# Attention on one core: shared block as two 64-column products, last rows padded to 128, products of one array shape issued together, low halves split a step later

## The reference

```python
def _attn_ref(q, k, v, tau):          # q, k, v: (4, 8, 576, 64) float32
    scale = 1.0 / np.sqrt(q.shape[-1])
    scores = scale * np.matmul(q, k.transpose(0, 1, 3, 2))
    thresh = np.max(scores, axis=-1, keepdims=True) - tau
    scores = np.where(scores >= thresh, scores, -1000000000.0)
    scores = scores - np.max(scores, axis=-1, keepdims=True)
    attn = np.exp(scores)
    attn = attn / (np.sum(attn, axis=-1, keepdims=True) + 1e-09)
    return np.matmul(attn, v).astype(np.float32)
```

## Time and profile before

| | |
|---|---|
| three runs | 1110.48, 1111.07, 1113.72 us; median 1111.07 |
| profiled execution | 1115.11 us; span of its instructions 1113.4 us |
| busy in the span | PE 94%, DVE 60%, ACT 50%, POOL 39% |
| attention part | to about 333 us of the span |
| TensorE's mean granted clock | 0.975 |

### The profile page before, as it was taken

How to read it: one execution, slowest core, us unless ns; L and a number is a source line. 1 busy time by engine, 2 the same in 40 slices (tenths; PEclk the granted TensorE clock), 3 DMA queues, 4 the chain that set the end, 5 groups by cost and what they waited for, 6 DMA issues and landing times. The chain is left out here.

```text
span 1113.4 us, 22407 instructions
## 1 busy us (share of the span) xinstructions
PE 1042.4 (94%) x8153; PEld 924.9 (83%) x8153; DVE 664.1 (60%) x1336; ACT 554.3 (50%) x854; POOL 432.9 (39%) x689
## 2 busy tenths in 40 slices
PE   7999999999989999999899989999379999999995
PEld 5778787787869999999899989999367777777774
DVE  5888787877855534343334333433567777777773
ACT  4777777777762311111111111111167888777772
POOL 4777777777750000000000000000147766667752
PEclk9999999999998999999999999999579999999998
DMA  4323223232203100000000000000782455511100
GB/s 107 80 60 82 53 66 80 63 81 51 53 2 115 39 20 1 25 1 20 3 25 1 20 2 24 1 20 1 277 322 112 166 197 183 190 38 39 39 28 22
DMA packets 76314, 75.40 MB, mean 68 GB/s; under 512 B 48815, under 2 KB 54959, under 8 KB 76210
## 3 DMA queue, kind: packets, MB, share of 16 engines
q1 hardware_dynamic: 72690, 63.49, 18.5%
q0 software_dynamic: 3520, 10.49, 2.8%
HBM read 64.52 MB, written 10.49 MB: 67 GB/s over the span
## 5 line engine op out<-in xcount | busy, mean ns | idle before, releaser
L820 ACT ACTIVATE r_buf<-h_ps 128x288 f32<-128x288 f32 x128 | 52.7, 412 | 348.2 <-PE h_ps L777 348.2
L884 DVE TENSOR_TENSOR r_buf<-r_buf 128x288 f32<-128x288 f32 x128 | 58.7, 459 | 244.4 <-ACT r_buf L820 244.4
L1156 POOL MEMSET ones<- 128x128 bf16 x1 | 0.2, 210 | 454.0 <-POOLq L637 454.0
L1322 ACT ACTIVATE w_hi<-w_experts 128x2048 fp32r x88 | 161.5, 1908 | 14.0 <-issue 14.0
L1093 DVE TENSOR_TENSOR w_lo<-w_experts,w_hi 128x2048 fp32r<-128x2048 f32 x66 | 149.5, 2292 | 28.0 <-ACT w_hi L1322 28.0
L777 PE MATMUL h_ps<-x_hi,w_in_hi 128*128 128x288 f32 x512 | 154.5, 302 | 6.6 <-DVE x_lo L878 3.5
L777 PE MATMUL h_ps<-x_hi,w_in_lo 128*128 128x288 f32 x512 | 151.9, 297 | 3.4 <-issue 3.4
L777 PE MATMUL h_ps<-x_lo,w_in_hi 128*128 128x288 f32 x512 | 152.5, 298 | 0.0
L796 PE MATMUL y_ps<-g_hi,w_out_hi 128*128 128x288 f32 x512 | 151.5, 296 | 0.3 <-DVE g_lo L890 0.3
L796 PE MATMUL y_ps<-g_hi,w_out_lo 128*128 128x288 f32 x512 | 151.3, 296 | 0.0
L796 PE MATMUL y_ps<-g_lo,w_out_hi 128*128 128x288 f32 x512 | 151.2, 295 | 0.0
(11 more groups left out here) (193 smaller groups left out, 2338.6 us busy)
## 6 DMA issues: line engine op xcount, KB each, us to landing
w_experts<-in_moe_w_dram SPq DMA_DIRECT2D x16, 2048.0 KB, 12.6
k_raw<-in_k_dram SPq DMA_DIRECT2D x32, 128.0 KB, 3.1
q_raw<-in_q_dram SPq DMA_DIRECT2D x32, 128.0 KB, 2.9
w_raw<-in_moe_w_in_dram SPq DMA_DIRECT2D x16, 256.0 KB, 3.2
v_nat<-in_v_dram SPq DMA_DIRECT2D x16, 256.0 KB, 2.6
y_T<-in_moe_w_out_dram SPq DMA_DIRECT2D x16, 256.0 KB, 2.7
y_rows<-y_row SPq DMA_DIRECT2D x16, 256.0 KB, 2.2
v_odd<-in_v_dram SPq DMA_DIRECT2D x16, 64.0 KB, 2.3
```

The costliest lines, as they stand in the source:

```text
L820: nc.scalar.activation(r_buf[f % 2][:], h_ps[f % 2][:, 0:HALF], ACT.Relu).then_inc(relu_done, 1)
L884: nc.vector.tensor_tensor(r[:], r[:], r[:], ALU.mult).then_inc(g_ops, 1)
L1156: nc.gpsimd.memset(ones[:], 1.0).then_inc(pool_set, 1)
L1322: nc.scalar.activation(group_of(w_hi, g), raw_group(buf, g), ACT.Copy).then_inc(hi_done, 1)
```

## The change

- The shared block is multiplied as two products of 64 columns (`v_mix[:, 0:D]` for the even head, `v_mix[:, D:2*D]` for the odd one), beside the four others: five pairs of half products and no full one.
- The last 64 rows are padded to 128: v's last rows lie in partitions 64 to 127 with zeros before them, k's last rows have zeros behind them, and the transposes and products of the tail and the ends use all 128 rows.
- `broadcast_rinv` (c = 1) and `output_tail` (now c = 3, one step later) are issued right behind `output_main`.
- The tail and the ends have columns of their own in `m_ps`; the wait for the tail's readers moves from `transposed_ends` to `transposed_k`.
- `q_hi` and `q_lo` move from c = 1 to c = 2, `ends_hi` and `ends_lo` from c = 3 to c = 4, the tail's copy and normalisation to c = 4. Orders within steps of ACT and DVE change with them; the reciprocal goes from the end of step 0 to behind the first maximum of step 1.

```diff
@@ attention: constants @@
+        SETUP = 12
+        TAIL_OUT, TAIL_R, Q_END, K_END = 0, TAIL, 2 * TAIL, 2 * TAIL + P
@@ load_v @@
-                sp.dma_start(v_nat[b][0:TAIL, :, LAST, :],
+                sp.dma_start(v_nat[b][TAIL:P, :, LAST, :],
@@ transposed_k @@
-                if i >= 1:
+                if i == 1:
+                    pe.wait_ge(klo_done, 1)
+                elif i >= 2:
                     pe.wait_ge(elo_done, 2 * i)
+                if i >= 3:
+                    pe.wait_ge(rbc_tail_done, i - 2)
+                    pe.wait_ge(x_tail_done, i - 2)
@@ transposed_ends @@
-                else:
-                    pe.wait_ge(rbc_tail_done, i - 1)
-                    pe.wait_ge(x_tail_done, i - 1)
-                pe.transpose(bank[:, 0:P], q_raw[b][:, LAST, :], ident[:])
-                pe.transpose(bank[:, P:P + TAIL], k_raw[b][0:TAIL, LAST, :], ident[0:TAIL, 0:TAIL]).then_inc(ends_set, 1)
+                pe.transpose(bank[:, Q_END:Q_END + P], q_raw[b][:, LAST, :], ident[:])
+                pe.transpose(bank[:, K_END:K_END + P], k_raw[b][:, LAST, :], ident[:]).then_inc(ends_set, 1)
@@ transposed_probs @@
-                    last = pe.transpose(out[0:TAIL, 0:P], probs[c][:, MAIN:S], ident[:])
+                    last = pe.transpose(out[:, 0:P], probs[c][:, S - P:S], ident[:])
@@ output_main @@
-                for kc in range(LAST):
-                    pe.matmul(o_ps[0:D, cols], v_nat[b][:, 0, kc, :], pt[:, kc, :], ...)
-                    pe.matmul(o_ps[D:P, cols], v_odd[b][:, kc, :], pt[:, LAST + 1 + kc, :], ...)
-                pe.matmul(o_ps[:, cols], v_mix[b][:], pt[:, LAST, :], start=False, stop=(c == LAST - 1),
-                          skip_group_check=True).then_inc(pv_done, 1)
+                for kc in range(QC):
+                    even = v_nat[b][:, 0, kc, :] if kc < LAST else v_mix[b][:, 0:D]
+                    odd = v_mix[b][:, D:2 * D] if kc == 0 else v_odd[b][:, kc - 1, :]
+                    pe.matmul(o_ps[0:D, cols], even, pt[:, kc, :], ...)
+                    last = pe.matmul(o_ps[D:P, cols], odd, pt[:, LAST + kc, :], ...)
+                last.then_inc(pv_done, 1)
@@ output_tail @@
-                    rows = P if kc < LAST else TAIL
-                        last = pe.matmul(m_ps[D * par:D * (par + 1), 0:TAIL], v_nat[b][0:rows, par, kc, :],
-                                  tail_T[0:rows, kc, par * TAIL:(par + 1) * TAIL], ...)
+                        last = pe.matmul(m_ps[D * par:D * (par + 1), TAIL_OUT:TAIL_OUT + TAIL], v_nat[b][:, par, kc, :],
+                                         tail_T[:, kc, par * TAIL:(par + 1) * TAIL], ...)
@@ TensorE's loop @@
-                if c == 1 and i >= 1:
-                    broadcast_rinv(i - 1)
                 if 0 <= made[0] < PAIRS:
                     for s in range(2):
                         transposed_probs(*made, s)
                 if c == 0 and i + 1 < PAIRS:
                     transposed_k(i + 1)
                 if 0 <= used[0] < PAIRS and used[1] < LAST:
                     output_main(*used)
+                if c == 1 and i >= 1:
+                    broadcast_rinv(i - 1)
+                if c == 3 and i >= 1:
+                    output_tail(i - 1)
                 if 0 <= made[0] < PAIRS and sets_in(made[1]) == 3:
                     transposed_probs(*made, 2)
                 if c == 1 and i + 1 < PAIRS:
                     transposed_q(i + 1)
-                if 0 <= used[0] and used[1] == LAST:
-                    output_tail(used[0])
                 if c == 3 and i + 1 < PAIRS:
                     transposed_ends(i + 1)
@@ ACT's copy_rinv_tail @@
+                if i + 2 < PAIRS:
+                    act.wait_ge(ends_set, i + 3)
@@ ACT's loop @@
+                if c == 2 and i + 1 < PAIRS:
+                    q_hi(i + 1)
+                if c == 4 and i >= 1:
+                    copy_rinv_tail(i - 1)
+                if c == 4 and i + 1 < PAIRS:
+                    ends_hi(i + 1)
                 if 0 <= made[0] < PAIRS:
                     for s in range(2):
                         evacuate(*made, s)
+                if c == 0 and i + 1 < PAIRS:
+                    k_hi(i + 1)
                 if i < PAIRS:
                     exponential(i, c, 0)
+                if c == 1 and i >= 1:
+                    copy_rinv(i - 1)
                 if 0 <= made[0] < PAIRS and sets_in(made[1]) == 3:
                     evacuate(*made, 2)
                 if i < PAIRS and len(heads_in(c)) == 2:
                     exponential(i, c, 1)
@@ DVE: setup @@
+                V.memset(v_nat[b][0:TAIL, :, LAST, :], 0.0).then_inc(setup_done, 1)
+                V.memset(k_raw[b][TAIL:P, LAST, :], 0.0).then_inc(setup_done, 1)
@@ DVE's loop, as it is after @@
+                if i < PAIRS:
+                    maximum(i, c, 0)
+                if c == 1 and i >= 1:
+                    reciprocal(i - 1)
+                if i < PAIRS and len(heads_in(c)) == 2:
+                    maximum(i, c, 1)
+                if c == 2 and i + 1 < PAIRS:
+                    q_lo(i + 1)
+                if c == 4 and i + 1 < PAIRS:
+                    ends_lo(i + 1)
                 if 0 <= before[0] < PAIRS:
                     for h in heads_in(before[1]):
                         mask(*before, h)
                 if c == 0 and i + 1 < PAIRS:
                     k_lo(i + 1)
+                if c == 2 and i >= 1:
+                    normalise_main(i - 1)
+                if c == 4 and i >= 1:
+                    normalise_tail(i - 1)
```

More of the change, by code:

```diff
@@ L383, in output_main @@
                     else:
-                        pe.wait_ge(setup_done, 8)
+                        pe.wait_ge(setup_done, SETUP)
                 pe.wait_ge(evac_done, set_no(i, c, 2) + 1)
                 pt, cols = probs_T[m % 2], slice(c * P, (c + 1) * P)
-                for kc in range(LAST):
[L388 to L391, removed]
-                pe.matmul(o_ps[:, cols], v_mix[b][:], pt[:, LAST, :], start=False, stop=(c == LAST - 1),
-                          skip_group_check=True).then_inc(pv_done, 1)
+                for kc in range(QC):
+                    even = v_nat[b][:, 0, kc, :] if kc < LAST else v_mix[b][:, 0:D]
+                    odd = v_mix[b][:, D:2 * D] if kc == 0 else v_odd[b][:, kc - 1, :]
+                    pe.matmul(o_ps[0:D, cols], even, pt[:, kc, :], start=(c == 0 and kc == 0),
+                              stop=(c == LAST - 1 and kc == LAST), skip_group_check=True)
+                    last = pe.matmul(o_ps[D:P, cols], odd, pt[:, LAST + kc, :], start=(c == 0 and kc == 0),
+                                     stop=(c == LAST - 1 and kc == LAST), skip_group_check=True)
+                last.then_inc(pv_done, 1)
             def broadcast_rinv(i):
@@ L416, in output_tail @@
                 for par in range(2):
-                    pe.matmul(m_ps[D * par:D * (par + 1), TAIL:2 * TAIL],
+                    pe.matmul(m_ps[D * par:D * (par + 1), TAIL_R:TAIL_R + TAIL],
                               rinv[:, CHUNKS - 1:CHUNKS].broadcast_to([P, D]),
@@ L420, in output_tail @@
                 for kc in range(QC):
-                    rows = P if kc < LAST else TAIL
                     for par in range(2):
-                        last = pe.matmul(m_ps[D * par:D * (par + 1), 0:TAIL], v_nat[b][0:rows, par, kc, :],
-                                  tail_T[0:rows, kc, par * TAIL:(par + 1) * TAIL], start=(kc == 0), stop=(kc == LAST))
+                        last = pe.matmul(m_ps[D * par:D * (par + 1), TAIL_OUT:TAIL_OUT + TAIL], v_nat[b][:, par, kc, :],
+                                         tail_T[:, kc, par * TAIL:(par + 1) * TAIL], start=(kc == 0), stop=(kc == LAST))
                 last.then_inc(tail_set, 1)
@@ L434, in _ @@
             scores(0, 0)
-            for step in range(STEPS * PAIRS + 3):
+            for step in range(STEPS * PAIRS + 4):
                 i, c = divmod(step, STEPS)
                 made, used = divmod(step - 2, STEPS), divmod(step - 3, STEPS)
-                if c == 1 and i >= 1:
-                    broadcast_rinv(i - 1)
                 if 0 <= made[0] < PAIRS:
@@ L470, in ends_hi @@
                 bank = qk_bank(i, "ends")
-                nc.scalar.activation(kT_hi[i % 2][:, MAIN:S], bank[:, P:P + TAIL], ACT.Copy).then_inc(ehi_done, 1)
-                nc.scalar.activation(qT_hi[i % 2][:, MAIN:MAIN + P], bank[:, 0:P], ACT.Copy, scale=SCALE).then_inc(ehi_done, 1)
+                nc.scalar.activation(kT_hi[i % 2][:, MAIN:S], bank[:, K_END:K_END + TAIL], ACT.Copy).then_inc(ehi_done, 1)
+                nc.scalar.activation(qT_hi[i % 2][:, MAIN:MAIN + P], bank[:, Q_END:Q_END + P], ACT.Copy,
+                                     scale=SCALE).then_inc(ehi_done, 1)
             def exponential(i, c, h):
@@ L493, in evacuate @@
                 else:
-                    out, src = tail_T[0:TAIL, LAST, :], src[0:TAIL, 0:P]
+                    out, src = tail_T[:, LAST, :], src[:, 0:P]
```

(14 more changed lines are left out.)

28 lines of the change are left out of this document (4 added, 24 removed).

## The result

The changed kernel takes 1120.87 us in the median of five runs, the kernel before 1111.07: a ratio of 1.0084, with a 95% interval of 1.0060 to 1.0108. I had forecast 1114.7 in a range of 1107 to 1122, slower with a chance of 0.50.

The account below looks back on a forecast made before the run. TensorE's queue was taken to bound the attention, other engines close behind. Savings of 1.2 us a pair against stalls of 0.87 and 0.64 left +0.33 a pair, +3.6 us overall: 1114.7 from 1111.07, range 1107 to 1122.

Parts of the forecast that it names:

- Stall A: At transposed_q in step 1: TensorE waits for ACT's copy of the reciprocal broadcast, 0.87 us, 14 times.
- Stall B: Second transpose set of step 3: TensorE waits for DVE's masks of chunk 1, queued behind q_lo, 0.64 us a pair.
- step 3: 4.82: Time from the start of scores 3 to scores 4, forecast to grow from 3.86 to 4.82 us.
- Wait C: Step 0: TensorE waits for a bank because POOL's bias for chunk 4 is late; 0.07 us, between 0 and 0.3.
- Savings by shape: TensorE, per pair: shared block 0.22, broadcast behind output_main 0.15 plus 0.22 waiting, tail 0.33, ends 0.28; 1.2 us together.
- The rival that the shape price is not saved: Transposes ahead of scores still pay an entry and 128-row tails cost more: +0.2 to 0.5 a pair, 1118 to 1122; chance 0.07.
- steps 4 and 0: Times from scores 4 to the next scores 0, and from scores 0 to scores 1: forecast 3.36 and 4.00 us.
- The sum: 20.04 against 19.71 us a pair, +0.33, x14 = +4.6; first pair -0.1, last pair -0.9; +3.6 us.
- The weight load: Load behind load_v on SP's queue might reach POOL late; mostly slack supposed, otherwise 1119 to 1124, chance 0.13.

Follow-up runs that it names:

- Experiment 5: The changed kernel with broadcast_rinv, its copy and the reciprocal back at their old places, all else kept; ratio to the kernel before 1.0006.
- Experiment 2: The changed kernel with normalise_main moved from the end of DVE's step 2 to the end of its step 1; ratio to the kernel before 1.0046.
- Experiment 3: The changed kernel with DVE's step 2 reordered to maxima, masks, normalisation, then q_lo; ratio to the kernel before 1.0088.
- experiment 7: The kernel before with the last rows padded to 128 and every order as before; ratio to the kernel before 0.9982.
- experiment 8: The kernel before with the padding alone and POOL's weight split of step 3 moved behind the biases of step 4; ratio to the kernel before 0.9951.
- experiment 4: The changed kernel with normalise_main at the end of DVE's step 1 and q_lo behind the masks in step 2; ratio to the kernel before 0.9962.
- experiment 9: The kernel before with padding, POOL's split moved a place later, and the shared block as two halves; ratio to the kernel before 0.9921.

## Why the prediction was right, and where it was short

- *Stall A*: right. The transposes start 1.74 after the broadcast's first record (I had 1.85), so the stall is 0.76 where I had 0.87; the profile puts 9.8 us of idle time on this wait. Taking it away gave 1.35 a pair: the 0.76, and 0.59 for the transposes, which now fill the masks' wait. Experiment 5 shows the stall from the other side: with its cover back, 0.37 less a pair in spite of one block more.
- *Stall B*: right in place, cause and size (second set at S2 + 4.67; step 3 shorter by 0.60 once the masks come first).
- *The step that failed* is the term "step 3: 4.82". I named the normalisation as queued behind the masks, and looked for who waits for DVE after it (the maxima of chunk 3), but not for who waits for the normalisation itself: `output_main` of chunk 0 needs `x_main_done`. Experiment 2 gives this wait 0.17 a pair. The other 0.14 of step 3 (5.13 less 4.82) no run takes apart; in the trace it is several small terms: the tail with its exit takes 0.82 (145.47 to 146.29) where I had 0.75, the transposes and the ends behind it 0.53 (146.29 to 146.82) where I had 0.50, the second set starts 0.02 later and takes 0.02 more, and I had rounded 4.84 to 4.82.
- *Wait C* was priced at 0.07 and did not occur in the changed kernel: step 0 is 3.95, 0.04 shorter than before. Experiment 3, where step 3 is 0.60 shorter and the wait appears, fits with step 3's length having covered it. The mechanism is real: 0.73 in experiment 3, 0.50 in experiment 7, gone in 8.
- *Savings by shape*: right in sign and kind, too high in what reaches the time. The shared block gives 0.12 of 0.22, block and padding together 0.47 of some 0.7. Part of the difference is price: in steps 3, 4 and 0 the shared block gives 0.04 each, not 0.055, and the padded tail 0.14, not 0.19. Part is cover: in step 1 the reciprocal takes the block's 0.04, and in step 3 of experiment 8 `output_main` starts 1.89 after S3 instead of 1.78, its transposes in the masks' wait, while the ends save 0.26 of the 0.28. The rival that the shape price is not saved would give the same time as measured (1118 to 1122), but not these steps: in the changed kernel steps 4 and 0, which have no stall, came out at 3.35 and 3.95 where I had 3.36 and 4.00.
- *The sum*: 14 x 0.20 more a pair is 2.8 us, and 3.6 + 2.8 is 6.4; the attention really ends 6.3 later. The rest, 2.2 us of the profiled executions and 3.5 us of the medians, lies in parts that the change does not touch, and the twelve traces show it with either kernel. That the loss came out clear of noise, and not on its edge as forecast, is owed to step 3 and to these parts together.
- *The weight load*: today's slack took it, as supposed. In the changed kernel it was waited for only twice, for 0.9 us in all between 40 and 300 us.

## What to carry to other kernels

Putting products of one shape together saves a fixed price a block, but each of them also carries a hand-over (a bank, a copy) whose cover was the work that stood between. List for every moved instruction who waits for it, not only what it waits for. When TensorE's step gets shorter, look at once at the chains of the small engines with the next smallest slack; an order that puts off-path work where its engine is idle can be worth as much as the shapes: here moving the normalisation and `q_lo` took 0.77 a pair (experiment 4), the shapes alone 0.47 (experiment 9). And where a wait has two possible causes, look at which of them ended last, with its usual delay, before believing the name beside it.

## What the runs showed of the hardware

A POOL subtraction of 128x128 took 0.46 us when it started before one of DVE's masks, and 0.97 to 0.99 when it started inside one; the mask behind it then took 1.00 to 1.01 instead of 0.81. In the kernel before, a mask that started 0.05 to 0.08 after the subtraction took 0.99 to 1.02; in experiment 4, where it starts 0.26 to 0.29 after it, it took 0.81. So the one that comes second is held up if it comes early enough, POOL by some 0.5 and DVE by 0.2. POOL's bias of one column shows it too: 0.3 clear of a mask, 0.8 inside one (141.67 and 145.70 in the changed kernel). The Trainium skill (SBUF — State Buffer, SBUF: two separate sides) says that the pair of ports that GpSimd shares with VectorE is an exclusive lock for a whole instruction, also for a VectorE operation with two SBUF inputs against a GpSimd one that reads SBUF. The traces agree on who is held up; that DVE is held for the whole of POOL's instruction they do not show, since the mask loses 0.2 of the subtraction's 0.46. I had not expected that the order of two starts decides over 0.5 us of a pair of 20: in the padded kernel the mask starts 0.14 ahead of the subtraction (184.43 and 184.57) in all steady pairs but one, and 0.15 behind it (106.34 and 106.19) in that one.
